# VectorE rounds the second of the first two weight tiles, and one warm-up product fewer, in a chained attention and two-MLP kernel

## The chip, the cores and the metric

The kernel runs on one core of one Trainium2 chip. The metric is the device time of one execution in microseconds (us). Before the change the median of three executions is 529.99 us (529.9 to 530.66).

## The reference

Three stages follow each other, all in float32.

1. Decayed linear attention over batch 2, 8 heads, 768 positions, head width 64, in blocks of 64 positions. Each block adds a masked product of its own queries, keys and values to a product of the queries with a running 64x64 state; the state is then scaled and updated.
2. `h = x @ w_in` (1536 x 512 by 512 x 2048), `g = max(0.01 h, h)`, `x = g @ w_out` (2048 x 512).
3. `a = x @ w1`, `b = x @ w2` (512 x 1024 each), `h = (a * b) @ w3` (1024 x 1024), `out = h @ w_out` (1024 x 512).

The kernel uses that the last two products of stage 3 have no function between them: it first multiplies `w3` by the last `w_out` and then needs one product by that result. This product of weights needs nothing of the attention, and it is the work with which TensorE begins.

## The kernel before, in words

**The numbers.** Every large product is made from operands split in two: a rounded part ("hi", in the type fp32r) and what is left of the exact value ("lo", also fp32r). A product is then three TensorE instructions: hi by hi, hi by lo, lo by hi (`product`, L987 to L991). A weight tile is 128 x 512 floats (256 KB). It takes four steps: SyncE issues its load from HBM into one of eight places of `stage` (`load_weight`, L405 to L418); ScalarE rounds it from `stage` into its hi place (`weight_hi`, L582 to L586, semaphore `hi_done`); VectorE subtracts the hi part from the exact tile in `stage` and writes the lo part (`weight_lo`, L775 to L778, through `lo_part`, L766, semaphore `split_done`); TensorE multiplies. The load of tile w+8 waits for the lo part of tile w, since it takes its place in `stage` (L408).

**The order.** `ORDER` lists all weight tiles. ScalarE and VectorE take them one after the other in this order, with the attention's work in between at places fixed by hand. The first 14 tiles (`EARLY_34`) are tiles of `w3` and of the last `w_out` in turns: tile 0 is `("w3", 0)`, tile 1 is `("wl", 0)`, tiles 2 and 3 are the next such pair, and so on. They lie in `wb`.

**The start on each engine.** SyncE issues the loads of tiles 0 to 7, then the queries and keys of chunk 0 (L430), tiles 8 and 9, the values of chunk 0 (L430), tiles 10 and 11, and after a wait the decay table (L444). GpSimd makes the powers of lambda (L481), and later scales keys (L491) and queries (L497) of each chunk. ScalarE issues two small loads, and then rounds tiles 0 to 13 in a plain loop (L609 to L612). VectorE clears `probs` (L768, a corner of `w_in_lo_place`), gives starting credits, and makes the lo parts of tiles 0 to 5 (L780, L781), two small copies (L783, L784) and the lo parts of tiles 6 to 13.

TensorE waits for the cleared `probs` and makes `WARM_UP` products of zeros into a bank that nobody reads (L1084 to L1086). Then comes its first useful work, `first_step` (L1089 to L1099), the first four 128x512 products of the weight product. It is ordered by when operands come: the four hi-by-hi instructions wait for both rounded tiles (L1090); the four with `w3`'s lo part wait for the lo part of tile 0 (L1093); the four with `wl`'s lo part wait for the lo part of tile 1 (L1096). Then the lambda powers are spread over the partitions (L1104, L1107), and `w34_products` (L993 to L1005) goes on with the later tiles, with the attention's chunks between (L1110 to L1116). After that come the large products of stages 2 and 3.

The lines of the wait and the first products are:

```python
            pe.wait_ge(hi_done, max(PLACE["w3", 0], PLACE["wl", 0]) + 1)
            for slot, cols in enumerate(first_step):
                nc.tensor.matmul(w34_acc[slot], w3(0)[0][:, cols], wl(0)[0], start=True, stop=False)
            pe.wait_ge(split_done, CREDIT_SPLIT + PLACE["w3", 0] + 1)
```

Of the kernel before, what the change touches and what calls it, by code (L numbers as in the profile page):

```python
# [45 lines left out]
POW_COPY_AFTER = 6  # L46


WARM_UP = 4

# [84 lines left out]
def weight_order():  # L137

    names = list(EARLY_34)
    for s in range(1, EARLY_CHUNKS + 1):  # L140
        names += segment_order(s)
    names += [("out", f) for f in range(W_OUT_AHEAD)]
    for f in range(F1):
        names += pass_order(f)
    for f in range(F1):
        names += last_pass_order(f)

    for f in range(1, F2):
        names += set_order("w12", f)
    for f in range(F2):  # L150
        names += set_order("again", f)
    return names
# [13 lines left out]
ORDER = weight_order()  # L166
PLACE = {name: w for w, name in enumerate(ORDER)}
# [6 lines left out]
def build(nc, attn, lam, head_selector, weights, outT):  # L174
    with ExitStack() as ctx:
# [3 lines left out]
        def sem(name):  # L179
            return ctx.enter_context(nc.semaphore(name))  # L180
# [100 lines left out]
        def set_slot(f, i):  # L281
            return FIRST_SET + SET * (f % 2) + i
# [16 lines left out]
        staged = [sem(f"staged{i}") for i in range(STAGE)]  # L299
# [9 lines left out]
        x_hi_done = sem("x_hi_done")  # L309
        x_split = sem("x_split")  # L310
        hi_done = sem("hi_done")
        split_done = sem("split_done")
        w34_done = sem("w34_done")
        w34_copied = sem("w34_copied")
# [34 lines left out]
        def w3(i):  # L349
            return wb[:, K34 + i % RING34, 0, :], wb[:, K34 + i % RING34, 1, :]  # L350
# [4 lines left out]
        def dest(name):  # L355

            kind, i = name
            if kind == "w3":
                return w3(i)
            if kind == "in":  # L360
                return wa_hi[:, i], wa_lo[:, i]
            if kind in ("w12", "again"):
                return wa_hi[:, set_slot(i // 2, i % 2)], wa_lo[:, set_slot(i // 2, i % 2)]
            return wb[:, i, 0, :], wb[:, i, 1, :]

        def staged_tile(w, like):

            tile = stage[:, w % STAGE, :]
            return tile.rearrange("p (k m) -> p k m", k=KD_TILES) if len(like.shape) == 3 else tile
# [181 lines left out]
        def _(act):  # L551
# [5 lines left out]
            def place_is_free(kind, i):  # L557
                if kind == "w3" and i >= RING34:
                    act.wait_ge(w34_done, HALF * (i - RING34 + 1))
                if kind == "out":  # L560
                    if i < K34:
                        act.wait_ge(w34_done, len(PRODUCTS) - HALF * (K34 - i - 1))
                    elif i < 10:
                        act.wait_ge(w34_done, len(PRODUCTS) - HALF * (K34 + RING34 - i - 1))
                    else:
                        place = [OUT_10, OUT_12, OUT_14][(i - 10) // 2]
                        act.wait_ge(chunk_done, NCHUNK - PLACES[::-1].index(place))
                if kind == "in" and i >= F1 - 2:
                    act.wait_ge(chunk_done, NCHUNK)
                if kind == "w34":  # L570
                    act.wait_ge(acc_done, CREDIT_G + 2 * F1 + i + 1)
                f = i // 2
                if kind == "w12" and f < 2:
                    act.wait_ge(hid_ready, 2 * F1 + FIRST_SET + SET * (f + 1))
                elif kind == "w12":
                    act.wait_ge(z_ready, 2 * (f - 1))
                elif kind == "again" and f < 2:
                    act.wait_ge(z_ready, 2 * (F2 - 1 + f))
                elif kind == "again":
                    act.wait_ge(hid_ready, N1 + f - 1)  # L580

            def weight_hi(w):  # L582
                place_is_free(*ORDER[w])
                act.wait_ge(staged[w % STAGE], 16 * (w // STAGE + 1))
                hi = dest(ORDER[w])[0]
                nc.scalar.copy(hi, staged_tile(w, hi)).then_inc(hi_done, 1)  # L586
# [21 lines left out]

            w = 0  # L609
            for _ in EARLY_34:  # L610
                weight_hi(w)
                w += 1  # L612
            for s in range(1, EARLY_CHUNKS + 1):
                if s > 1:
# [149 lines left out]
        def _(dve):  # L764
            def lo_part(out, exact, hi, done):
                nc.vector.tensor_tensor(out, exact, hi.bitcast(F32), ALU.subtract).then_inc(done, 1)  # L766
# [6 lines left out]
            dve.sem_inc(y_split, CREDIT_ACC)  # L773

            def weight_lo(w):  # L775
                dve.wait_ge(hi_done, w + 1)
                hi, lo = dest(ORDER[w])
                lo_part(lo, staged_tile(w, lo), hi, split_done)  # L778

            for w in range(POW_COPY_AFTER):  # L780
                weight_lo(w)  # L781
            dve.wait_ge(pow_spread, 1)
# [2 lines left out]
            for w in range(POW_COPY_AFTER, len(EARLY_34)):  # L785
                weight_lo(w)
# [71 lines left out]
            w = len(EARLY_34)  # L858
            for s in range(1, EARLY_CHUNKS + 1):
                mask(s - 1)  # L860
                update_states(s - 1)
                if s > 1:
                    x_lo(s - 2)
                for _ in segment_order(s):
                    weight_lo(w)
                    w += 1
# [117 lines left out]
        def _(pe):  # L984
# [99 lines left out]
            pe.wait_ge(zeroed, 1)  # L1084
            for _ in range(WARM_UP):
                nc.tensor.matmul(hid[:, 0, 0, 0:2 * P], probs[:, 0, 0:2, :], probs[:, 0, :, :], start=True, stop=True)  # L1086


            first_step = [slice(slot * P, (slot + 1) * P) for slot in range(HALF)]  # L1089
            pe.wait_ge(hi_done, max(PLACE["w3", 0], PLACE["wl", 0]) + 1)  # L1090
            for slot, cols in enumerate(first_step):
                nc.tensor.matmul(w34_acc[slot], w3(0)[0][:, cols], wl(0)[0], start=True, stop=False)
            pe.wait_ge(split_done, CREDIT_SPLIT + PLACE["w3", 0] + 1)  # L1093
# [252 lines left out]
```

## Time and profile before

| what | value |
|---|---|
| median of three executions | 529.99 us (529.9, 529.99, 530.66) |
| the profiled execution | 530.02 us |
| its span, first to last instruction | 528.2 us |
| TensorE busy with matmuls | 522.9 us (99% of the span) |
| VectorE busy | 261.7 us (50%) |
| ScalarE busy | 172.1 us (33%) |
| GpSimd busy | 92.4 us (18%) |
| DMA | 43.85 MB, mean 83 GB/s |

How to read it: the span runs from the first instruction's start to the last one's end; the execution's own time is 1.82 us longer than its span. PE is TensorE's matmuls and PEld its weight loads, which overlap them; DVE is VectorE, ACT ScalarE, POOL GpSimd, SPq the queue in which SyncE issues transfers. A matmul's record holds its way through the array, so consecutive records overlap, and their pace is told by the distance of their starts. A float32 product shows as two matmul records, a product of fp32r operands as one.

### The profile page before, as it was taken

Reading aid. Unit: us, or ns where it says so; the run is one execution under the profiler, and the core shown is the slowest. Engines: PE = TensorE matmul, PEld = TensorE weight load, DVE = VectorE, ACT = ScalarE, POOL = GpSimd, SP = SyncE. Lnnn points to the kernel's source line nnn. Section 1 sums busy time; section 2 is a strip of 40 time slices with the busy share of each in tenths; the row PEclk is TensorE's granted clock in tenths of the full one; section 3 lists DMA queues with packets and bytes.
Section 4 is the critical chain, followed back from the end, with each engine's and each line's share of the span. In section 5 each row is a group of like instructions: output and inputs, shape, how many; then the busy total and the mean of one; then the engine's idle time right before and its main releaser. Section 6 shows DMA issues by size and latency. Waiting matters only on the chain.

```text
span 528.2 us, 9088 instructions
## 1 busy us (share of the span) xinstructions
PE 522.9 (99%) x3652; PEld 431.3 (82%) x3652; DVE 261.7 (50%) x387; ACT 172.1 (33%) x299; POOL 92.4 (18%) x89
## 2 busy tenths in 40 slices
PE   8999999999999999999999999999999999999997
PEld 6888888888888888888888888888888888888885
DVE  4677355655543222222334687487777653322332
ACT  5353333343333212222322334442222214232221
POOL 2223131122000000000003992222222200000000
PEclk9999999999999999999999999999999999999999
DMA  8999483441310000000001111011111111105002
GB/s 288 333 369 329 165 276 103 160 158 47 120 60 21 0 1 0 0 1 0 1 0 42 60 41 60 22 38 62 41 42 40 41 40 40 41 14 187 0 1 79
DMA packets 22344, 43.85 MB, mean 83 GB/s; under 512 B 3344, under 2 KB 3352, under 8 KB 22304
## 3 DMA queue, kind: packets, MB, share of 16 engines
q1 hardware_dynamic: 19824, 35.66, 19.8%
q10 hardware_dynamic: 2448, 7.62, 4.3%
q8 instruction: 29, 0.48, 0.4%
q14 instruction: 11, 0.09, 0.1%
q0 software_dynamic: 32, 0.00, 0.0%
HBM read 38.03 MB, written 5.25 MB: 82 GB/s over the span
## 4 chain that ended last, share of the span: by engine, by line
PE 99%; ACT 0%; DVE 0%; issue 0%; DVEq 0%
PE acc L989 14%; PE acc L991 14%; PE acc L990 14%; PE hid L989 13%; PE hid L991 12%; PE hid L990 12%; PE hid L1211 5%; PE hid L1210 5%; PE hid L1209 5%; PE hid L1021 1%; PE hid L1036 1%; PE hid L1049 1%; PE hid L1060 1%; PE hid L1086 1%; PE acc L1060 0%; PE acc L1049 0%
## 5 line engine op out<-in xcount | busy, mean ns | idle before, releaser
L989 PE MATMUL acc<-g_hi,wb 128*128 128x512 f32 x286 | 111.7, 391 | 0.0
L991 PE MATMUL acc<-g_hi,wb 128*128 128x512 f32 x286 | 111.3, 389 | 0.0
L990 PE MATMUL acc<-g_lo,wb 128*128 128x512 f32 x286 | 111.3, 389 | 0.0
L989 PE MATMUL hid<-xy_hi,wa_hi 128*128 128x512 f32 x256 | 100.0, 391 | 0.0
L991 PE MATMUL hid<-xy_hi,wa_lo 128*128 128x512 f32 x256 | 99.6, 389 | 0.0
L990 PE MATMUL hid<-xy_lo,wa_hi 128*128 128x512 f32 x256 | 99.6, 389 | 0.0
L840 DVE TENSOR_TENSOR g<-g,hid 128x512 f32<-128x512 f32 (+1 forms) x48 | 33.0, 687 | 102.4 <-ACT g L634 102.3
L634 ACT ACTIVATE g<-hid 128x512 f32<-128x512 f32 (+1 forms) x48 | 28.7, 598 | 128.4 <-PE hid L991 128.4
L766 DVE TENSOR_TENSOR g_lo<-g,g_hi 128x512 fp32r<-128x512 f32 (+1 forms) x64 | 50.4, 788 | 39.7 <-ACT g_hi L640 32.9
L989 PEld LDWEIGHTS acc<-g_hi,wb 128*128 128x128 f32 x286 | 53.7, 188 | 11.2
L990 PEld LDWEIGHTS acc<-g_lo,wb 128*128 128x128 f32 x286 | 53.7, 188 | 11.2
L991 PEld LDWEIGHTS acc<-g_hi,wb 128*128 128x128 f32 x286 | 53.7, 188 | 11.1
L989 PEld LDWEIGHTS hid<-xy_hi,wa_hi 128*128 128x128 f32 x256 | 48.1, 188 | 10.1
L991 PEld LDWEIGHTS hid<-xy_hi,wa_lo 128*128 128x128 f32 x256 | 48.0, 188 | 10.0
L990 PEld LDWEIGHTS hid<-xy_lo,wa_hi 128*128 128x128 f32 x256 | 48.0, 188 | 9.9
L766 DVE TENSOR_TENSOR wb<-stage,wb 128x512 fp32r<-128x512 f32 x48 | 38.7, 824 | 10.7 <-ACT wb L586 10.7
L640 ACT CAST g_hi<-g 128x512 fp32r<-128x512 f32 (+1 forms) x48 | 29.8, 621 | 41.1 <-DVE g L840 41.1
L586 ACT CAST wb<-stage 128x512 fp32r<-128x512 f32 x48 | 29.7, 621 | 20.2 <-DMA stage<-weights 14.6
L766 DVE TENSOR_TENSOR wa_lo<-stage,wa_hi 128x512 fp32r<-128x512 f32 x48 | 34.4, 749 | 0.0
L512 POOL TENSOR_TENSOR w_in_lo_place<-xy_hi 128x512 f32<-128x512 f32 x2 | 3.0, 1512 | 155.6 <-PE hid L991 155.6
L586 ACT CAST wa_hi<-stage 128x512 fp32r<-128x512 f32 x48 | 27.9, 620 | 0.1
L672 ACT CAST g_hi<-g 128x512 fp32r<-128x512 f32 x16 | 9.9, 621 | 52.2 <-DVE g L949 44.8
(135 smaller groups left out, 639.1 us busy)
## 6 DMA issues: line engine op xcount, KB each, us to landing
stage<-weights SPq DMA_DIRECT2D x88, 256.0 KB, 3.4
w_out_place<-attn ACTq DMA_DIRECT2D x12, 512.0 KB, 4.8
outT<-x_hi_place SPq DMA_DIRECT2D x11, 256.0 KB, 3.2
x_hi_place<-attn SPq DMA_DIRECT2D x4, 512.0 KB, 8.8
w_out_place<-attn SPq DMA_DIRECT2D x4, 512.0 KB, 7.6
w_dram<-x_lo_place SPq DMA_DIRECT2D x8, 256.0 KB, 5.4
stage<-w_dram SPq DMA_DIRECT2D x8, 256.0 KB, 2.9
x_lo_place<-attn SPq DMA_DIRECT2D x2, 512.0 KB, 6.2
```

The source lines that it names most:

```text
L586: nc.scalar.copy(hi, staged_tile(w, hi)).then_inc(hi_done, 1)
L634: nc.scalar.mul(g[:, n % 2, :], source, factor).then_inc(scaled, 1)
L640: nc.scalar.copy(g_hi[:, n % 2, :], g[:, n % 2, :]).then_inc(g_hi_done, 1)
L672: nc.scalar.copy(g_hi[:, n % 2, :], source).then_inc(g_hi_done, 1)
L766: nc.vector.tensor_tensor(out, exact, hi.bitcast(F32), ALU.subtract).then_inc(done, 1)
L840: nc.vector.tensor_tensor(g[:, n % 2, :], g[:, n % 2, :], source, ALU.max).then_inc(g_ready, 1)
L989: nc.tensor.matmul(out, w_hi, a_hi, start=first, stop=False)
L990: nc.tensor.matmul(out, w_hi, a_lo, start=False, stop=False)
L991: return nc.tensor.matmul(out, w_lo, a_hi, start=False, stop=final)
L1209: nc.tensor.matmul(out, w_hi, a_hi, start=first and row == 0, stop=False, skip_group_check=True)
L1210: nc.tensor.matmul(out, w_hi, a_lo, start=False, stop=False, skip_group_check=True)
L1211: last = nc.tensor.matmul(out, w_lo, a_hi, start=False, stop=row == 1, skip_group_check=True)
```

## The change

`WARM_UP` goes from 4 to 3. The rounding of tile 1 moves from ScalarE to VectorE, in front of VectorE's first lo part, and reports to a semaphore of its own, `first_hi_done`. ScalarE, in place of that rounding, only adds one to `hi_done`, so that the counts of all later tiles stay as they were. VectorE's lo part of tile 0 waits for `hi_done` at 2, that of tile 1 for `first_hi_done`. TensorE's first product waits for both semaphores.

```diff
-WARM_UP = 4
+WARM_UP = 3
+DVE_ROUNDS = 1
...
+        first_hi_done = sem("first_hi_done")
...
             w = 0
             for _ in EARLY_34:
-                weight_hi(w)
+                if w == DVE_ROUNDS:
+                    act.sem_inc(hi_done, 1)
+                else:
+                    weight_hi(w)
                 w += 1
...
             def weight_lo(w):
-                dve.wait_ge(hi_done, w + 1)
+                if w == DVE_ROUNDS:
+                    dve.wait_ge(first_hi_done, 1)
+                else:
+
+                    dve.wait_ge(hi_done, w + 1 + (w < DVE_ROUNDS))
                 hi, lo = dest(ORDER[w])
                 lo_part(lo, staged_tile(w, lo), hi, split_done)
 
+            dve.wait_ge(staged[DVE_ROUNDS], 16)
+            hi = dest(ORDER[DVE_ROUNDS])[0]
+            nc.vector.tensor_copy(hi, staged_tile(DVE_ROUNDS, hi)).then_inc(first_hi_done, 1)
             for w in range(POW_COPY_AFTER):
                 weight_lo(w)
...
-            pe.wait_ge(hi_done, max(PLACE["w3", 0], PLACE["wl", 0]) + 1)
+            pe.wait_ge(hi_done, 2)
+            pe.wait_ge(first_hi_done, 1)
```

## Rows read from the trace of the kernel before

**Rows 1.** The page: engine shares, and the chain that ended last, by engine.
```profile
PE 522.9 (99%) x3652; PEld 431.3 (82%) x3652; DVE 261.7 (50%) x387; ACT 172.1 (33%) x299; POOL 92.4 (18%) x89
...
PE 99%; ACT 0%; DVE 0%; issue 0%; DVEq 0%
```

**Rows 2.** The chain that ended last in order of time, 0 to 20 us: start, length, what.
```profile
0.93 0.50 DVE w_in_lo_place L768
...
1.47 3.71 PE hid L1086 x8
5.18 0.49 PE hid L1092 x2
...
7.97 1.03 PE acc L1104 x8
...
9.22 0.43 PE hid L989
```

**Rows 3.** TensorE in order of time: start, length, line, [idle before].
```profile
3.76 1.06 PE L1086 MATMUL hid<-w_in_lo_place 128*128 128x256 f32 x2
...
4.62 0.56 PE L1086 MATMUL hid<-w_in_lo_place 128*128 128x256 f32 x1
4.93 0.50 PE L1092 MATMUL hid<-wb 128*128 128x512 f32 x1
...
4.93 0.19 PEld L1092 LDWEIGHTS hid<-wb 128*128 128x128 f32 x1 [0.40 <-ACT wb L586]
...
5.51 0.63 PE L1092 MATMUL acc<-wb 128*128 128x512 f32 x2
...
7.36 0.61 PE L1098 MATMUL acc<-wb 128*128 128x512 f32 x2
7.91 1.10 PE L1104 MATMUL acc<-g 8*128 8x64 f32 x8
8.94 0.28 PE L1107 MATMUL acc<-g 8*64 8x8 f32 x4
9.15 0.50 PE L989 MATMUL hid<-wb 128*128 128x512 f32 x1
```

**Rows 4.** ScalarE's first roundings and VectorE's lo parts, in order of time.
```profile
3.52 0.62 ACT L586 CAST wb<-stage 128x512 fp32r<-128x512 f32 x1 [0.46 <-DMA stage<-weights]
...
4.26 0.62 ACT L586 CAST wb<-stage 128x512 fp32r<-128x512 f32 x1
...
6.74 0.62 ACT L586 CAST wb<-stage 128x512 fp32r<-128x512 f32 x1 [1.86 <-DMA stage<-weights]
...
7.38 0.62 ACT L586 CAST wb<-stage 128x512 fp32r<-128x512 f32 x1
...
4.17 0.69 DVE L766 TENSOR_TENSOR wb<-stage,wb 128x512 fp32r<-128x512 f32 x1 [2.75 <-ACT wb L586]
...
4.91 0.69 DVE L766 TENSOR_TENSOR wb<-stage,wb 128x512 fp32r<-128x512 f32 x1
...
7.39 0.69 DVE L766 TENSOR_TENSOR wb<-stage,wb 128x512 fp32r<-128x512 f32 x1 [1.79 <-ACT wb L586]
...
8.04 0.69 DVE L766 TENSOR_TENSOR wb<-stage,wb 128x512 fp32r<-128x512 f32 x1
```

**Rows 5.** The staging tile, 1.2 to 1.3 us: the load of tile 1.
```profile
L418 SPq DMA_DIRECT2D stage<-weights x1: 424/424/424, 1.2 to 1.2; - x1
...
DMA to landing us min/median/max: 3.0/3.0/3.0
```

**Rows 6.** VectorE's groups by line: duration in ns min/median/max, start, form.
```profile
L768 DVE MEMSET w_in_lo_place<- x1: 485/485/485, 0.9 to 0.9; 128x512 f32 x1
...
L980 DVE COPY x_hi_place<-acc x2: 691/692/692, 523.3 to 524.0; 128x512 f32<-128x512 f32 x2
...
L783 DVE COPY k_pow<-acc x1: 159/159/159, 10.0 to 10.0; 128x8 f32<-128x8 f32 x1
```

**Rows 7.** Weight loads of TensorE by line, same columns as rows 6.
```profile
L1086 PEld LDWEIGHTS hid<-w_in_lo_place x8: 287/337/337, 1.5 to 4.2; 128*128 128x128 f32 x8
...
L1104 PEld LDWEIGHTS acc<-g x8: 181/187/187, 7.9 to 8.7; 8*128 8x128 f32 x8
```

**Rows 8.** Stretches: length, busy us (x) of PE, PEld, DVE, ACT, POOL, then PEclk, DMA share, GB/s.
```profile
1.47:5.00 3.53, 3.53 (x9) 2.59 (x9) 0.78 (x2) 2.52 (x3) 1.71 (x4) 1.00 0.86 254
5.00:9.20 4.20, 4.20 (x26) 3.32 (x25) 2.41 (x4) 2.37 (x4) 1.84 (x3) 1.00 1.01 341
9.20:30.00 20.80, 20.80 (x254) 17.08 (x253) 15.16 (x24) 9.16 (x16) 4.75 (x4) 1.00 1.02 349
```

**Rows 9.** SyncE's queue in order of time: start, length, line.
```profile
4.51 0.66 SPq L430 DMA_DIRECT2D x_hi_place<-attn  x1
...
5.29 0.60 SPq L418 DMA_DIRECT2D stage<-weights  x1
...
6.01 0.36 SPq L418 DMA_DIRECT2D stage<-weights  x1
...
6.42 0.64 SPq L430 DMA_DIRECT2D x_hi_place<-attn  x1
...
8.17 0.33 SPq L418 DMA_DIRECT2D stage<-weights  x1
```

**Rows 10.** What waits for transfers between 10 and 25 us, and its readers on TensorE.
```profile
14.80 1.04 POOL L491 TENSOR_TENSOR x_hi_place<-x_hi_place,k_pow 128x512 f32<-128x512 f32 x1 [7.52 <-DMA x_hi_place<-attn]
...
18.05 0.65 PE L1036 MATMUL hid<-x_hi_place 64*64 64x64 f32 x32
...
13.25 1.32 DVE L766 TENSOR_TENSOR wb<-stage,wb 128x512 fp32r<-128x512 f32 x2 [1.61 <-ACT wb L586]
...
18.62 0.50 PE L989 MATMUL hid<-wb 128*128 128x512 f32 x1
```

**Rows 11.** The waits of the whole span that name TensorE as the waiting engine.
```profile
PEld hid L1049 <- issue: 2.8, 8, 0.4
...
PE hid L1086 <- DVE w_in_lo_place L768: 1.5, 1, 1.5
...
PEld hid L989 <- issue: 1.0, 2, 0.5
PEld hid L1092 <- ACT wb L586: 0.4, 1, 0.4
```

## The prediction

> **What bounds the kernel now.** I read the page first. TensorE is busy for 99% of the span and the chain that ended last is TensorE's for 99% [rows 1], so the kernel is as long as TensorE's work, plus the time before its first useful product, plus the tail. The list of waits says the same: over the whole span TensorE is stopped by another engine only for the memset ahead of the warm-up (1.5 us, the start itself), and its weight load once for 0.4 us by ScalarE's rounding; the rest are gaps of its own issue [rows 11]. So what the change can give is what it takes off the start of the first product L1092, as long as no later operand is then late.
>
> I then read the chain in order of time [rows 2] and TensorE's own rows [rows 3]. The warm-up runs from 1.47 to a modelled 5.18 us. The first product's record starts at 4.93, behind ScalarE's second rounding, which ends at 4.26 + 0.62 = 4.88 [rows 4]: from its end to TensorE's start a signal takes 0.05 us. The record overlaps the last warm-up record, so I ask when the array is really free for it. From L1092's third product to L1098's third, eight products take 7.36 - 5.51 = 1.85 us, 0.231 each. The third starts at 5.51; two places back is 5.05. That is the working start of the useful work. The last warm-up record starts at 4.62, and such records follow each other every 0.43 us (3.76, then 4.62 two later), so the warm-up streams until 4.62 + 0.43 = 5.05. Two things thus end almost together: the warm-up at 5.05, ScalarE's second rounding at 4.93 with its signal. Taking away either alone would give at most 0.1 us; the change takes away both.
>
> **The clock at the start.** The profile grants 1.00 in all three stretches [rows 8]; but in the warm-up a float32 load of 128 columns takes 337 ns and at L1104 187 ns [rows 7], and the warm-up's pace is 256 columns of a two-record product in 0.43 us. So I take the granted clock's row as silent on the first microseconds, the warm-up as running at the lower level of the two (1.2 GHz), and the rise to 2.4 GHz as falling at the end of the warm-up: L1092's first record is 0.50 us, the third and fourth 0.63 together [rows 3]. I take 4.98 for the rise, between the first record's start and the 5.05 above.
>
> **The change part by part.**
>
> *One warm-up product fewer.* It is two records of 0.43 us, so the stream ends at 5.05 - 0.86 = 4.19. It is then no bound: nothing useful is ready before.
>
> *Tile 0.* ScalarE still rounds it from 3.52 to 4.14 [rows 4]; with the signal 4.19. ScalarE's bare increment for tile 1 is issued behind it and costs nothing: the next rounding waits for a transfer until 6.74 anyway. The 0.62 us that ScalarE saves is idle time.
>
> *Tile 1 on VectorE.* Its load was issued at 1.2 and landed 3.0 us later, at 4.2 [rows 5]; ScalarE started it at 4.26, 0.12 us after its first rounding, where two ready ones follow in 0.02 (6.74 + 0.62 = 7.36, then 7.38 [rows 4]). So it was the landing that released it, and VectorE, idle since 1.4, can start at 4.24. The trace has no VectorE copy from SBUF to SBUF. Its nearest rows [rows 6]: a copy of the same shape out of PSUM, 0.692 us; the memset of the same shape, which writes SBUF only, 0.485; and an 8-column copy, 0.159, which is the fixed part and a floor. A two-operand subtraction from SBUF takes 0.69 [rows 4], a ceiling that agrees with the first. I take 0.485: it is the only VectorE row of this shape that touches SBUF with at most one operand. The ends are 0.16 and 0.69. Done at 4.24 + 0.49 = 4.73, with the signal TensorE starts at 4.78; at the ends 4.45 and 4.98.
>
> The Trainium skill ("VectorE: DVE Perf Modes", The perf-mode tier table) says that a float32 `tensor_copy` between SBUF tiles runs at twice the rate of `tensor_tensor`, while any PSUM operand caps it; its timings would make the copy about 0.33 to 0.42 us, an estimate from that page, and the start 4.62 to 4.71. No row here shows it, and the sum below would gain another 0.04 to 0.08 us.
>
> *The second wait on TensorE.* It is one more instruction ahead of L1092, while TensorE is idle from 4.19 to 4.78; it lies there. The trace shows no wait alone; the signal of 0.05 is my bound for it, 0 to 0.05, and I take 0.
>
> *What the earlier start is worth.* From 4.78 to 4.98 the array would still run at half pace, so those 0.20 us do 0.10 us of work. The start is worth one at 4.98 - 0.10 = 4.88, against 5.05 before: **0.17 us gained**. With the slow copy 5.05 - 4.98 = 0.07, less up to 0.05 for the extra wait: 0.02. With the fast one, 0.53 us at half pace: 5.05 - (4.98 - 0.265) = 0.335.
>
> *What is late next.* VectorE's lo part of tile 0 moves behind the copy: 4.75 to 5.44 (before 4.17 to 4.86). TensorE asks for it after four products, at 4.88 + 4 x 0.231 = 5.80: 0.3 us to spare; with the slow copy it ends at 5.65 and is asked for at 5.90. The lo part of tile 1 ends at 6.16, asked for at 6.7. Then VectorE is idle until 7.39 as before, for tile 2 comes by transfer [rows 4]. The lo part of tile 3 ends at 8.04 + 0.69 = 8.73, and L989 starts at 9.15 [rows 3, 4]: less the signal, 0.37 us to spare. This is the cap of what the start can give, just above my upper end.
>
> *The queues.* SyncE's load of tile 8 waits for the lo part of tile 0, tile 9's for that of tile 1 [rows 9]. Tile 8 was issued at 5.29, 0.12 us after L430 was through; with the lo part at 5.44 it goes out at about 5.5, tile 9 at 6.2 to 6.4 for 6.01, and behind it chunk 0's values at 6.6 to 6.8 for 6.42. Tile 10 waits for tile 2's lo part, at 8.17 as before. The transfers' share is 1.0 in this stretch [rows 8], so landings follow the bytes in the queue more than the issue; at worst they are 0.4 us later. The values free L491 at 14.80, which ends at 15.84, and TensorE reads at 18.05: 2.2 us to spare. Tiles 8 and 9 have their lo parts at 14.57 and are asked for at 18.62: 4 us [rows 10]. Nothing of this comes through. GpSimd's and ScalarE's queues have nothing moved.
>
> **Sum.** 530.02 - 0.17 = 529.85, say 529.8, us for the profiled execution. It lies 0.03 above the median of 529.99, so the median goes to 529.8 as well. A measurement of this kernel tells 0.2% from no change, that is 1.06 us (below 528.93 or above 531.05); the three executions of before alone spread over 0.76.
>
> **The rivals.**
>
> *No earlier start (529.95).* The copy is as slow as one from PSUM, or the second wait costs its 0.05; the gain is 0.02 to 0.07. For it: two of three rows of this shape say 0.69. Against: they read PSUM or two operands. Here the change does half of what it says: VectorE rounds beside ScalarE, but ends no earlier than ScalarE would have.
>
> *The clock rises later (about 531.5, slower).* Before, TensorE streamed without a break from 1.47 into the useful work, and the rise came at the end of the warm-up. Now it stops at 4.19 for about 0.6 us. Every product that runs at the lower level costs another 0.23 us. Between none and all twelve of the first step I price seven: 7 x 0.231 = 1.62 lost, less 0.17, so 531.5. It is slower by over 1.06 once (1.06 + 0.17) / 0.231 = 5.3 products are caught: from the sixth on. For it: the rise comes just as the fourth warm-up product ends, with nothing to spare, and a product is now missing from exactly there. Against: TensorE is still busy for most of that stretch, and the profile grants 1.00 through the small products of L1104 and L1107, with much less in the array [rows 8]. The Trainium skill ("TensorE: Matmul & The Clock Gate", Part 1) says that the throttled state is the default, that activity releases it, and that the point of release varies from run to run with a phase that the kernel does not set. By that rule part of the 0.76 us between the executions of before is this, and the change could come out on either side by as much.
>
> *A larger gain (529.65).* The copy takes 0.3 us or less, and the rise doesn't come later; capped at 0.37 by tile 3's lo part.
>
> *A late transfer.* It would need landings 2.2 us later for 0.4 us later issues; I see no way to it.
>
> **How the numbers follow.** Forecast (gain about 0.1 to 0.25): 0.60. No earlier start: 0.19. The clock later: 0.13, of which 0.10 beyond the bound. A larger gain: 0.06. A late transfer: 0.02. Range: 529.3 (the larger gain's 529.65 less half of the executions' spread) to 531.0 (the forecast's slow end 529.95 plus that spread of 0.76 and part of the late clock); beyond it lies most of the late clock and little else. Faster by over 0.2% would need four times the cap, and has only what I don't see: 0.03. Slower 0.10. Within 0.2%: 0.87.
>
> **What the changed profile would show.** L1086 as six records, ending near 4.3. A VectorE COPY `wb<-stage` from about 4.24, of 0.33 to 0.69 us. L1092 starting 0.05 us after it, with the wait put down to VectorE. L766's first lo part near 4.75. L989 near 8.97 for 9.15. Weight loads of L1092 at about 190 ns if the clock rose as before, and near 340 well past 5 us if not. No TensorE wait on a transfer or on L766 before 30 us. The prediction is wrong if L1095 or L989 waits for L766, if the pace of L1095 is over 0.3 us a product, or if the span changes by more than 1 us with none of these.

## The result and the profile after

The changed kernel takes 531.32 us (median of 14 executions, 529.37 to 531.92), the kernel before 529.99 (median of 14, 529.46 to 530.66): 1.33 us slower. The ratio of the mean times is 1.002, with a 95% interval of 1.0011 to 1.003. That is clear of the noise, if only just, and outside the range of 529.3 to 531.0 that was forecast. The 14 times fall in two groups: three of 529.37 to 530.25, which are as before, and eleven of 531.02 to 531.92. The profiled execution is of the second group, at 531.14 us with a span of 529.3.

TensorE in order of time, first 12 us of the changed kernel (start, length, line):

```profile
1.47 2.93 PE L1098 MATMUL hid<-w_in_lo_place 128*128 128x256 f32 x6 [1.47 <-DVE w_in_lo_place L773]
5.18 1.19 PE L1105 MATMUL hid<-wb 128*128 128x512 f32 x2 [0.78 <-DVE wb L791]
6.17 1.05 PE L1105 MATMUL acc<-wb 128*128 128x512 f32 x2
7.02 1.05 PE L1108 MATMUL hid<-wb 128*128 128x512 f32 x2
7.87 1.05 PE L1108 MATMUL acc<-wb 128*128 128x512 f32 x2
8.73 0.68 PE L1111 MATMUL hid<-wb 128*128 128x512 f32 x2
9.25 0.63 PE L1111 MATMUL acc<-wb 128*128 128x512 f32 x2
9.81 1.10 PE L1117 MATMUL acc<-g 8*128 8x64 f32 x8
10.84 0.28 PE L1120 MATMUL acc<-g 8*64 8x8 f32 x4
11.05 0.51 PE L1001 MATMUL hid<-wb 128*128 128x512 f32 x1
```

Against [rows 3]: pairs of the first step's products, which had records of 0.63 us and starts 0.46 apart, now have records of 1.05 and starts 0.85 apart, so one product per 0.43 us, until 8.73 us. From then on they are at 0.63 again. L1117 starts at 9.81 (L1104 before: 7.91) and L1001 at 11.05 (L989 before: 9.15), both 1.90 later. TensorE's weight loads by line (ns min/median/max, and when they started) say the same; compare 337 and 187 ns in [rows 7]:

```profile
L1108 PEld LDWEIGHTS hid<-wb x2: 330/330/330, 6.6 to 7.0; 128*128 128x128 f32 x2
...
L1111 PEld LDWEIGHTS hid<-wb x2: 240/285/330, 8.3 to 8.7; 128*128 128x128 f32 x2
...
L1111 PEld LDWEIGHTS acc<-wb x2: 187/188/188, 9.0 to 9.2; 128*128 128x128 f32 x2
```

The same load takes 330 ns until about 8.7 us and 188 after 9.0. In the kernel before that step lay at about 5 us. So eight of the twelve products of the first step ran at the lower level of the clock.

VectorE, ScalarE and SyncE at the start of the changed kernel:

```profile
4.61 0.43 DVE L791 CAST wb<-stage 128x512 fp32r<-128x512 f32 x1 [3.19 <-DMA stage<-weights]
4.95 0.68 DVE L771 TENSOR_TENSOR wb<-stage,wb 128x512 fp32r<-128x512 f32 x1
...
3.65 0.62 ACT L588 CAST wb<-stage 128x512 fp32r<-128x512 f32 x1 [0.60 <-DMA stage<-weights]
5.05 0.62 ACT L588 CAST wb<-stage 128x512 fp32r<-128x512 f32 x1 [0.78 <-DMA stage<-weights]
...
5.74 0.92 SPq L420 DMA_DIRECT2D stage<-weights  x2
6.70 0.43 SPq L432 DMA_DIRECT2D x_hi_place<-attn  x1
```

VectorE's rounding takes 0.43 us, against the 0.485 that was taken. It starts at 4.61 instead of 4.24, since tile 1 landed later in this execution, and TensorE starts 0.14 us after it ends, not 0.05. ScalarE's second row is tile 2, which came at 5.05 here and at 6.74 before: landings differ by that much between the traces. The loads behind the lo parts go out 0.3 to 0.45 us later than in [rows 9], about as worked out, and nothing on TensorE's path waits for them: GpSimd's L493 starts at 14.64 (14.80 in [rows 10]).

```profile
14.64 1.04 POOL L493 TENSOR_TENSOR x_hi_place<-x_hi_place,k_pow 128x512 f32<-128x512 f32 x1 [6.63 <-DMA x_hi_place<-attn]
```

The loss at L1001 is 1.90 us, but the span grew by 1.1 only. The waits of TensorE after the start show where 0.7 to 0.8 us came back; first the changed kernel, between 9.6 and 140 us (total, times, longest):

```profile
PEld hid L1061 <- issue: 2.8, 8, 0.4
PEld hid L1033 <- issue: 1.8, 5, 0.4
...
PEld hid L1061 <- PE hid L1072: 0.2, 1, 0.2
```

The kernel before had one more such row, `PEld hid L989 <- issue: 1.0, 2, 0.5` [rows 11]. The timeline has its two places:

```profile
32.06 0.19 PEld L989 LDWEIGHTS hid<-wb 128*128 128x128 f32 x1 [0.49 <-issue]
...
48.47 0.19 PEld L989 LDWEIGHTS hid<-wb 128*128 128x128 f32 x1 [0.48 <-issue]
```

TensorE's matmul starts are 0.34 us further apart than their pace at the first place, and 0.32 at the second. The kernel before stood still there; the changed kernel, 1.9 us later, did not.

### The profile page after: what moved, and what is told of

It is laid out like the page before. It is cut to its first block, busy times and chain, and to the rows that moved or that the text cites. A ratio compares the mean times of both kernels' runs of the same rounds, so it can differ in the third digit from the quotient of the medians.

```text
span 529.3 us, 9086 instructions
## 1 busy us (share of the span) xinstructions
PE 523.5 (99%) x3650; PEld 432.1 (82%) x3650; DVE 260.6 (49%) x388; ACT 171.6 (32%) x298; POOL 93.2 (18%) x89
## 4 chain that ended last, share of the span: by engine, by line
PE 98%; DMA 1%; ACT 0%; DVE 0%; SPq 0%; issue 0%
PE acc L1001 14%; PE acc L1002 14%; PE acc L1003 14%; PE hid L1001 13%; PE hid L1002 12%; PE hid L1003 12%; PE hid L1222 5%; PE hid L1223 5%; PE hid L1224 5%; PE hid L1033 1%; PE hid L1048 1%; PE hid L1061 1%; PE hid L1072 1%; DMA stage<-weights 1%; PE acc L1072 0%; PE acc L1061 0%
## 5 line engine op out<-in xcount | busy, mean ns | idle before, releaser
L1001 PE MATMUL acc<-g_hi,wb 128*128 128x512 f32 x286 | 111.7, 391 | 0.0
L1002 PE MATMUL acc<-g_lo,wb 128*128 128x512 f32 x286 | 111.3, 389 | 0.0
L1001 PE MATMUL hid<-xy_hi,wa_hi 128*128 128x512 f32 x256 | 100.0, 391 | 0.0
L1002 PE MATMUL hid<-xy_lo,wa_hi 128*128 128x512 f32 x256 | 99.6, 389 | 0.0
L1001 PEld LDWEIGHTS acc<-g_hi,wb 128*128 128x128 f32 x286 | 53.7, 188 | 11.3
L1002 PEld LDWEIGHTS acc<-g_lo,wb 128*128 128x128 f32 x286 | 53.7, 188 | 11.0
L1001 PEld LDWEIGHTS hid<-xy_hi,wa_hi 128*128 128x128 f32 x256 | 48.1, 188 | 10.1
L1002 PEld LDWEIGHTS hid<-xy_lo,wa_hi 128*128 128x128 f32 x256 | 48.0, 188 | 9.8
```

The lines of the kernel that those rows point to most:

```text
L1001: nc.tensor.matmul(out, w_hi, a_hi, start=first, stop=False)
L1002: nc.tensor.matmul(out, w_hi, a_lo, start=False, stop=False)
```

## The experiments

Two theories were set against each other first. The **clock theory**: the missing warm-up product leaves a pause, and the rise comes after the useful work has begun. The **rival**: VectorE's rounding, the lo parts behind it and the delayed loads cost the time. Before-times differ a little between groups of runs (medians 530.16, 530.01 and 530.25); each run is compared with the kernel before of its own group. Of these 88 executions of the kernel before, eight took over 531.0 us, so it has a slow tail too.

**VectorE's rounding alone.**

```diff
 # the changed kernel
-WARM_UP = 3
+WARM_UP = 4
```

> VectorE rounds tile 1, but four warm-up products stay. Clock theory (the change loses because the rise of TensorE's clock comes later once a warm-up product is missing): as the kernel before, 529.9, at most 0.1 us less; the warm-up ends at 5.05, the first useful product starts behind it, and all twelve products of the first step but the first start about 0.23 us apart. Rival (VectorE's rounding, the later lo parts and the later loads behind them cost the time): as the changed kernel, about 531.3, with the clock risen early.

530.36 against 530.16, ratio 1.0004 (0.9995 to 1.0013): no loss beyond the noise, as the clock theory expected. The profiled execution, at 531.02 one of its slowest, has the fast pace from the start, and is long for another reason:

```profile
5.07 0.79 PE L1105 MATMUL hid<-wb 128*128 128x512 f32 x2
5.70 0.63 PE L1105 MATMUL acc<-wb 128*128 128x512 f32 x2
...
32.63 0.47 PE L1001 MATMUL hid<-wb 128*128 128x512 f32 x1 [0.45 <-ACT x_lo_place L596]
...
49.45 0.19 PEld L1001 LDWEIGHTS hid<-wb 128*128 128x128 f32 x1 [0.92 <-issue]
```

The same two places as before, with longer stalls.

**The missing product alone.**

```diff
 # the kernel before
-WARM_UP = 4
+WARM_UP = 3
```

> The kernel before with three warm-up products and nothing else. Clock theory: about 531.3 like the changed kernel, with six to nine of the first products 0.43 us apart. Rival (VectorE's rounding and the queues): 529.9, since the first product starts at 4.93 as before.

531.6 against 530.16, ratio 1.0019 (1.0002 to 1.0036, from six executions): the whole loss, with ScalarE still rounding both tiles. In its trace ten of the twelve products are slow:

```profile
4.90 1.22 PE L1092 MATMUL hid<-wb 128*128 128x512 f32 x2 [0.50 <-ACT wb L586]
...
8.48 1.05 PE L1098 MATMUL hid<-wb 128*128 128x512 f32 x2
9.33 0.89 PE L1098 MATMUL acc<-wb 128*128 128x512 f32 x2
...
11.39 0.50 PE L989 MATMUL hid<-wb 128*128 128x512 f32 x1
```

The two runs together settle which half of the change costs: the missing product.

**Three products later, with ScalarE's rounding.**

```diff
 # the kernel before, WARM_UP = 3
-            nc.vector.memset(probs[:, :, :, :], 0.0).then_inc(zeroed, 1)
+            for again in range(3):
+                if again:
+                    dve.wait_ge(zeroed, again)
+                nc.vector.memset(probs[:, :, :, :], 0.0).then_inc(zeroed, 1)
...
-            pe.wait_ge(zeroed, 1)
+            pe.wait_ge(zeroed, 3)
```

> The kernel before with three warm-up products that start about 0.9 us later (the memset ahead of them is made three times), so that they end where the four ended, with no pause before the first useful product. If the pause delays the rise: as before, 529.9. If it is the time since TensorE began, or the number of products: as the changed kernel, 531.3 or near it. Rival (VectorE's rounding): 529.9.

530.76 against 530.16, ratio 1.0009 (1.0 to 1.0018): between the two, and not a clean test. The waits between the memsets cost 0.17 us each, so that the warm-up streamed until about 5.5 (2.78 and six records of 0.43, plus 0.14 as in the kernel before), later than meant. In the profiled execution tile 1 came late too: ScalarE rounded it from 5.15 to 5.77, and the first useful product started at 5.82, behind a pause of some 0.3 us:

```profile
2.78 2.93 PE L1089 MATMUL hid<-w_in_lo_place 128*128 128x256 f32 x6 [2.78 <-DVE w_in_lo_place L771]
5.82 1.22 PE L1095 MATMUL hid<-wb 128*128 128x512 f32 x2
```

**Half a product more.**

```diff
 # the changed kernel, after the warm-up loop
+            nc.tensor.matmul(hid[:, 0, 0, 0:P], probs[:, 0, 0:2, :], probs[:, 0, 0:2, :], start=True, stop=True)
```

> The changed kernel with a half product (128 columns, 0.43 us) behind the three warm-up products, which ends at about 4.62, before VectorE's rounding is through. Clock theory: nearly no pause, the clock rises mostly as before, 529.8, or a median between that and 531.3 if the pause left over still matters in some executions. Rival: 531.3.

530.22 against 530.16, ratio 1.0001 (0.9992 to 1.001). A product of 0.43 us gives the whole loss back at the end. Its trace shows that the start is not as before, though:

```profile
6.65 0.90 PE L1109 MATMUL hid<-wb 128*128 128x512 f32 x2
7.40 0.63 PE L1109 MATMUL acc<-wb 128*128 128x512 f32 x2
```

The slow pace lasted until about 7.3 us, and L1001 started at 10.12, 0.97 later than before. The span is only 0.2 us longer, because there were no stalls later.

**The pause by itself.** This is the clean form of the test: the same three products and VectorE's rounding, moved so that the warm-up ends when the rounding does.

```diff
 # the changed kernel
-            nc.vector.memset(probs[:, :, :, :], 0.0).then_inc(zeroed, 1)
+            for again in range(2):
+                if again:
+                    dve.wait_ge(zeroed, again)
+                nc.vector.memset(probs[:, :, :, :], 0.0).then_inc(zeroed, 1)
...
-            pe.wait_ge(zeroed, 1)
+            pe.wait_ge(zeroed, 2)
```

> The changed kernel with its three warm-up products moved 0.66 us later (the memset ahead of them made twice), so that they end about when VectorE's rounding does: the same three products, the same first useful product, and no pause between them. If the pause is what delays the rise of the clock: 529.9 to 530.3. If it is that one product is missing, or how early TensorE begins: as the changed kernel, 531.3 or a little more.

530.44 against 530.25, ratio 1.0003 (0.9993 to 1.0014). The warm-up is as short as in the changed kernel and begins later, and yet most of the loss is gone:

```profile
2.13 2.93 PE L1101 MATMUL hid<-w_in_lo_place 128*128 128x256 f32 x6 [2.13 <-DVE w_in_lo_place L776]
4.70 1.22 PE L1108 MATMUL hid<-wb 128*128 128x512 f32 x2
5.71 1.06 PE L1108 MATMUL acc<-wb 128*128 128x512 f32 x2
6.56 0.80 PE L1111 MATMUL hid<-wb 128*128 128x512 f32 x2
7.20 0.62 PE L1111 MATMUL acc<-wb 128*128 128x512 f32 x2
```

The slow pace ends at about 6.9 us here, and at about 8.8 in the changed kernel, with as many products in the warm-up. So most of the lateness is the pause's. It is not shown that the number of products has no part in the rest, from 5 us to 6.9.

**What a later start costs.** Two kernels hold TensorE longer before the useful work.

```diff
 # the kernel before; the second with 6
-WARM_UP = 4
+WARM_UP = 5
```

> The kernel before with five warm-up products: the first useful product starts at 5.91 instead of 5.05, with the clock risen by then in nearly every execution. It measures what a start 0.86 us later costs at the end. Theory A (two stalls of TensorE of 0.34 us near 32 us and 0.32 us near 48 us in the kernel before, which end at times that the start doesn't set, swallow a later start): 0.2 us at the end, 530.2, and no such stalls in its trace. Theory B (a delay at the start reaches the end whole): 530.9, the stalls still there. Both: a narrower spread than before, since the clock can't rise late.

> The kernel before with six warm-up products: TensorE is held until about 5.9 to 6.8 whatever the clock, and the clock rises before the useful work. If a start 0.7 to 1.0 us later is swallowed by the stalls near 32 and 48 us (as in three traces so far): 0.2 to 0.5 us at the end, 530.2 to 530.5, and its trace has neither stall. If a start delay reaches the end whole: 530.8 to 531.8 with the stalls still there.

Five products: 530.3 against 530.01, ratio 1.0008 (0.9999 to 1.0017). The median fits the expected 530.2, but not its trace: the clock had risen before the warm-up ended, which cut it short, the useful work began at 5.03, and both stalls are there. Six products: 531.19 against 530.25, ratio 1.0017 (1.0006 to 1.0027). The expectation that the stalls swallow a later start had 530.2 to 530.5 and misses. L989 starts at 10.53, 1.38 later than in [rows 3], the stall near 32 us is gone, and one of 0.25 us lies near 48:

```profile
6.25 0.81 PE L1092 MATMUL hid<-wb 128*128 128x512 f32 x2
...
10.53 0.50 PE L989 MATMUL hid<-wb 128*128 128x512 f32 x1
...
48.65 0.13 PEld L1049 LDWEIGHTS acc<-w_in_lo_place,w_in_hi_place 64*64 64x64 f32 x1 [0.25 <-issue]
```

A later start is thus swallowed only as far as stalls are there to swallow it, by 0.3 us here and 0.8 in the changed kernel, and the rest reaches the end.

**A warm-up that begins earlier.** The memset ahead of it is made in halves, and the warm-up waits for the first.

```diff
 # the changed kernel, WARM_UP = 4
-            nc.vector.memset(probs[:, :, :, :], 0.0).then_inc(zeroed, 1)
+            for b in range(2):
+                nc.vector.memset(probs[:, b, :, :], 0.0).then_inc(zeroed, 1)
```

> The changed kernel with four warm-up products, and the memset ahead of them in two halves, of which they wait for the first, so that they start and end about 0.2 us earlier (4.85) and the first useful product follows VectorE's rounding with no pause. Clock theory: the rise is as early as before, 0 to 0.2 us gained at L1001's start, and by theory A (the stalls near 32 and 48 us) nothing of it at the end: 529.9 to 530.2. By theory B the gain comes through: 529.8 to 529.9. If VectorE's rounding cost time by itself: 530.5 or more.

529.87 against 530.01, ratio 0.9997 (0.9988 to 1.0006): within the noise of before, and the lowest median of all versions. In its trace the warm-up begins at 1.20 and the rise still comes late, at about 7.1, after four slow products; L1001 starts at 10.13, but with no stall later.

**The stall near 32 us.** ScalarE's program has a cause for it: it rounds tile 20, which it must wait for, ahead of the copies that free the banks.

```diff
 # the kernel before
-                    if tile == COPY_BEFORE[0]:
+                    if tile == ("w3", K34 + RING34 - 2):
                         copy_w34(0)
```

> The kernel before with ScalarE's copies of the first four weight products moved ahead of its rounding of tile 20, which waits for a transfer until 30.84 us. Theory A: the stall near 32 us goes (0.34 us), but the one near 48 us ends when it did, so the median falls by 0 to 0.3: 529.7 to 530.1, and the stall near 48 us is up to 0.66 long. Theory B (the stall near 32 us is the profile's own or is TensorE's issue): it stays, 530.1.

> Both of the two above together: VectorE's rounding, four warm-up products that start earlier, and the copies ahead of the rounding of tile 20. If the stall near 48 us ends at its own time: as the better of the two alone. If the stalls are independent: 0.2 to 0.5 us less than before, 529.6 to 529.9.

The first is slower, 530.83 against 530.01, ratio 1.0022 (1.0009 to 1.0035), where 0 to 0.3 us less was expected. The stall near 32 us is gone. ScalarE's rows, first of the kernel before, then with the copies first:

```profile
30.84 0.62 ACT L586 CAST wb<-stage 128x512 fp32r<-128x512 f32 x1 [2.35 <-DMA stage<-weights]
31.37 1.06 ACT L594 COPY x_lo_place<-hid 128x512 f32<-128x512 f32 x2
```

```profile
29.88 1.27 ACT L594 COPY x_lo_place<-hid 128x512 f32<-128x512 f32 x2 [1.67 <-PE hid L991]
...
48.37 0.19 PEld L989 LDWEIGHTS hid<-wb 128*128 128x128 f32 x1 [0.87 <-issue]
```

But the stall near 48 us has grown from 0.48 to 0.87: TensorE came earlier to a place that opened when it did before. This explains why nothing was gained, and not the 0.8 us that the median lost: the profiled execution took 529.89, the fastest of its eleven, and none of the others was traced. The second kernel, 530.96 against 530.01, ratio 1.0018 (1.0005 to 1.0032), was profiled in an execution of 533.44 us, far above its median. TensorE near 48 us, then the stretches (length, busy of PE, PEld, DVE, ACT, POOL, PEclk, DMA share, GB/s):

```profile
47.73 0.39 PE L1003 MATMUL hid<-wb 128*128 128x512 f32 x1
50.37 0.59 PE L1004 MATMUL hid<-wb 128*128 128x512 f32 x1 [2.25 <-issue]
50.76 0.63 PE L1002 MATMUL hid<-wb 128*128 128x512 f32 x1
```

```profile
47.00:50.00 3.00, 1.12 (x34) 0.81 (x27) 2.12 (x5) 1.04 (x2) 2.42 (x2) 1.00 0.93 323
50.00:53.40 3.40, 3.03 (x8) 2.34 (x8) 3.37 (x6) 1.72 (x4) 0.08 (x1) 0.50 0.81 270
```

TensorE stands still for 2.25 us, no semaphore in the program is between these two matmuls of one product, and the granted clock is at 0.50 from 50.0 us, before the stall ends, to 53.4. The eight products from 50.37 to 53.61 cost 1.4 us more by it than at a pace of 0.23 each. Before the stall one packet of queue q8, "instruction", starts between 48 and 49 us. The answer for that microsecond:

```profile
DMA packets 152, 0.29 MB, mean 287 GB/s; under 512 B 19, under 2 KB 19, under 8 KB 151
...
q8 instruction: 1, 0.02, 5.8%
```

That TensorE waits here for its own code is supported by a count. The two rows below are the stretches from 0 to the end of the stall, in the kernel before and in the one with six warm-up products. The second entry with a count is PEld's, the weight loads that had started by then:

```profile
0.00:48.46 48.46, 46.86 (x599) 37.56 (x599) 31.11 (x51) 22.16 (x37) 13.04 (x21) 1.00 0.97 335
```

```profile
0.00:48.64 48.64, 47.06 (x599) 38.50 (x599) 29.75 (x49) 21.96 (x36) 12.39 (x20) 1.00 0.95 331
```

In all six traces with a stall near 48 us the first load after it is the 600th of the program, though it stands in L989 in two of them and in L990, L1049, L1001 and L1002 in the others. Five or six warm-up products move the stall to other work, and not to another count. The 600th load starts 2.2 to 2.6 us after the first q8 packet past 44 us in these six (46.17 to 48.47 in the kernel before, 48.11 to 50.38 in this one), and 2.7 to 4.9 us after it in the eight traces without the stall. So the packet is no sign of a stall by itself: TensorE stands still when it comes to that count too soon after it. No run changed the code's loading alone, so this stays inferred, though no data or semaphore of the program would keep to a count.

**A second look at either kernel**, unchanged.

> The changed kernel once more, for where its clock rises in another execution and what of a late start its later stalls give back. Clock theory: a rise anywhere from 5 to 10 us, L1001 at 9.0 us plus half of the time that the rise lies behind 5 us, and the span longer by that less about 0.7 us, with no stall near 32 and 48 us where L1001 starts after 10 us.

> The kernel before once more. Clock theory: a rise between 4.5 and 8 us, and the earlier it is the longer the stalls near 32 and 48 us, so that the time stays within 529.2 to 530.7.

The changed kernel took 531.46 us, its slow pace lasted until about 9.4 us, L1001 started at 11.29, and there were no stalls later. The kernel before took 529.59 with L989 at 9.43 and, against the expectation, neither stall: in that execution tile 20 was there at 30.15 instead of 30.84.

```profile
30.15 0.62 ACT L586 CAST wb<-stage 128x512 fp32r<-128x512 f32 x1 [1.55 <-DMA stage<-weights]
```

Its q8 packet came at 45.14 instead of 46.17. So the stalls are a matter of the execution, by when transfers land, and not a fixed part of the kernel before.

**All traces together.** The first L989 (L1001) is the first product after the first step. The slow pace's end is where the trace has the clock at its upper level for the first time; the distances of the matmuls' starts agree. Span less the start of L989:

| kernel | slow pace until | L989 starts | span | difference | stalls near 32, near 48 us |
|---|---|---|---|---|---|
| before | 5.0 | 9.15 | 528.2 | 519.0 | 0.49, 0.48 |
| before, second look | 4.8 | 9.43 | 527.8 | 518.4 | none |
| changed | 8.8 | 11.05 | 529.3 | 518.3 | none |
| changed, second look | 9.4 | 11.29 | 529.7 | 518.4 | none |
| VectorE's rounding, four products | 5.3 | 9.34 | 529.2 | 519.9 | 0.85, 0.92 |
| before with three products | 9.9 | 11.39 | 529.8 | 518.4 | none |
| three products later, ScalarE | 7.6 | 10.87 | 529.2 | 518.3 | none |
| changed, with half a product | 7.3 | 10.12 | 528.4 | 518.3 | none |
| changed, products later | 6.9 | 9.92 | 528.3 | 518.4 | none |
| VectorE, four, in halves | 7.1 | 10.13 | 528.4 | 518.3 | none |
| five products | 4.4 | 9.25 | 528.5 | 519.3 | 0.70, 0.44 |
| six products | 6.1 | 10.53 | 529.3 | 518.8 | none, 0.25 |
| before, copies first | 4.8 | 9.04 | 528.1 | 519.1 | none, 0.87 |
| VectorE, in halves, copies first | 5.7 | 9.46 | 531.6 | 522.1 | none, 2.45 |

(Stalls as idle time before a weight load, which in the kernel before is some 0.15 us more than what the matmuls lose.) Without stalls the kernel is its start plus 518.3 to 518.4 us, in every version. Five of the six traces that start by 9.5 us have a stall, and one of the eight later ones, of 0.25 us. The three traces with a pause of 0.7 to 1.0 us between warm-up and work have the slow pace until 8.8 to 9.9 us, the eleven others until 4.4 to 7.6.

## Why the prediction was wrong, point by point

**The bound.** Right that TensorE's start and TensorE's work make the span. Wrong that nothing else did: [rows 11] held 1.0 us in two stalls before L989, and the text called them gaps of TensorE's own issue. One of them, near 32 us, was ScalarE waiting for a transfer ahead of a copy that TensorE needed: the stall went when the copies were moved, in both kernels that did it. The argument that no later operand is late was made up to 18.6 us and taken for the rest.

**The step that failed: the clock.** The text took the rise to stay at 4.98 us and gave the late rise 0.13. It said against it that TensorE was busy for most of the stretch. The runs show that the pause decides: with it the rise came at 8.8 to 9.9 us and the medians are 531.3 and 531.6; without it 530.2 to 530.4, with the same three products or half a product more. In the profiled execution the pause was longer than forecast, from about 4.2 to 5.18 us: 0.37 of it came from tile 1's landing and 0.09 from the signal, less 0.06 for the faster copy. So the forecast start of 4.78 was 5.18, later than the 4.93 of before.

**The rival's price.** It had named the mechanism and 531.5; measured 531.32. Two of its terms were off, in opposite directions. A product at the lower level costs 0.43 - 0.23 = 0.20 us more, not 0.231, and eight were caught, not seven: 1.6 us. With the useful work beginning 0.26 later (the third product starts at 6.17, two places of 0.43 back is 5.31, against 5.05) that is the 1.90 at L1001, to within 0.05. And 0.8 came back at the end, 0.7 of it where the stalls of before had been. That 531.5 lies so near 531.32 is in part luck: the later useful work and the swallowed loss, both left out of it, went against each other. The mechanism was seen, and its chance mis-set: by their times, eleven executions of fourteen had it.

**The copy on VectorE.** Taken as 0.485 with ends of 0.16 and 0.69, measured 0.43 in every trace that has it. The Trainium skill's rule ("VectorE: DVE Perf Modes", The perf-mode tier table), by which it would be 0.33 to 0.42, comes nearer, at its upper end. **The second wait and the signal** were taken as 0.05 together; from the copy's end to TensorE's start are 0.14 us in this trace.

**Next in line.** None of the lo parts was waited for by TensorE, as forecast, but they came at other times than worked out. Tile 0's ran from 4.95 to 5.63, 0.2 later than forecast, and tile 1's until 6.23. Tile 3's, the cap of the forecast, ended at 8.01 instead of 8.73, since its transfer came earlier in this execution, and L1001 asked for it 1.9 us later than before. So the cap of 0.37 us was not put to the test.

**The earlier start's worth.** No run shows the 0.17 us, and none excludes it. VectorE's rounding with four products (530.36 against 530.16) kept the product that ends at 5.05. With the warm-up started earlier the times are 529.87 against 530.01, and the interval, of -0.6 to +0.3 us, holds both nothing and the 0.17; in its trace the rise was late and the start with it. By the table an earlier start would reach the end in an execution without stalls, and be lost in one that has them.

**What stays open.** Where exactly the clock rises in a given execution: the second look of either kernel has it elsewhere, and with four products from 1.20 on it came at 7.1 us in one kernel and at 5.7 in the one that also moves the copies, with four from 1.47 on at about 5. The Trainium skill ("TensorE: Matmul & The Clock Gate", Part 1) says that this point varies with a phase that the kernel doesn't set; the rises in the table and the two groups of times of the changed kernel agree with it, though no execution of the faster group was traced. Open too is what makes the q8 packet come at 46 us in one execution and at 48 in another, and why the median of the kernel with the copies first is 0.8 us higher.

## What to carry to other kernels

A warm-up isn't there to fill time until the operands come; it must run into the useful work without a pause, and a product of it that ends a little behind the operands costs some 0.1 us (5.05 against 4.93 in the kernel before, an estimate) where a pause of 0.7 to 1.0 us costs 1.3 to 1.4. Before an earlier start is counted as a gain, every idle entry of the bounding engine must be followed to what released it, the "issue" ones too, because a stage further on that opens at its own time takes the gain back. And a stall that stays at the same count of instructions when the work around it is moved is not to be looked for in the semaphores.

## What the runs showed of the hardware that was not expected

After a pause of TensorE of 1.0 us, behind 2.7 us of products, the clock stayed at its lower level for another 3.6 us of work in the changed kernel. In a stall of 2.25 us in the middle of dense work it fell from 1.00 to 0.50, for the stretch of 50.0 to 53.4 us. A matmul stream stood still for 0.25 to 2.45 us near 48 us in six traces of fourteen, each time before its 600th weight load, which started 2.2 to 2.6 us after a packet of the instruction queue. And with another stall removed in front of that place, the stall there grew from 0.48 to 0.87 us.
